# Two mixtures of experts behind an attention: rounds of 256 gathered tokens in place of slots of 128 sorted ones, and a result that stays in sorted order

## What is computed

```python
logits = xn @ en.T / tau                      # x and expert embeddings, normalised
expert_idx = np.argmax(logits, axis=1)
gate_w = probs[np.arange(N), expert_idx]      # softmax of logits, at the chosen expert
for e in range(8):                            # first mixture, w1[e] 512x1024, w2[e] 1024x512
    mask = expert_idx == e
    h = np.maximum(x[mask] @ w1[e], 0.0)
    out[mask] = gate_w[mask, None] * (h @ w2[e])
# second mixture, on that out; p = domain_probs / its row sum
for e in range(4):
    h = np.maximum(x @ w1[e], 0.0)
    out += p[:, e:e + 1] * (h @ w2[e])
```

## Time and profile before

| | us |
|---|---|
| three runs | 908.07, 909.2, 913.29 |
| median | 909.2 |
| profiled execution, its own time | 910.04 |
| its span (first to last instruction) | 908.2 |
| mean granted TensorE clock | 0.987 |

### The profile page before, as it was taken

The page is one execution under the profiler, slowest core; times in us unless marked ns, Lnnn a source line. Parts: engine busy times, 40 slices in busy tenths (PEclk is TensorE's granted clock), DMA queues, the critical chain, the costliest instruction groups (busy, mean ns, idle before and its releaser), DMA issues.

```text
span 908.2 us, 12900 instructions
## 1 busy us (share of the span) xinstructions
PE 860.9 (95%) x4433; PEld 695.1 (77%) x4434; DVE 300.3 (33%) x776; ACT 221.3 (24%) x476; POOL 288.8 (32%) x162
## 2 busy tenths in 40 slices
PE   7999945999999999999999999999999999999998
PEld 5666623788888788788888888888888888888886
DVE  6777770444444443223121212121212121211212
ACT  4878750033333323311111111111111111111010
POOL 4462613057777778630000650000830001400000
PEclk9999976999999999999999999999999999999999
DMA  6899623146666667620000230000320000001001
GB/s 246 265 315 342 221 78 140 31 124 213 205 204 205 195 220 220 174 94 1 1 0 0 70 116 0 0 0 0 115 71 0 0 0 0 1 0 46 29 17 46
DMA packets 33075, 90.96 MB, mean 100 GB/s; under 512 B 4232, under 2 KB 4616, under 8 KB 33040
## 3 DMA queue, kind: packets, MB, share of 16 engines
q1 hardware_dynamic: 23056, 54.86, 18.1%
q10 hardware_dynamic: 8064, 29.36, 10.6%
q0 software_dynamic: 1920, 6.29, 2.2%
HBM read 72.67 MB, written 17.83 MB: 100 GB/s over the span
## 4 chain that ended last, share of the span: by engine, by line
PE 84%; DMA 8%; DVE 3%; issue 2%; POOL 2%; SPq 1%; ACT 1%; DVEq 0%; ACTq 0%
PE ps L1209 29%; PE ps L1196 29%; PE ps L1153 10%; PE ps L1135 7%; DMA win<-qkv 3%; DMA xg<-x_sorted 3%; PE ps L1008 2%; PE ps L1034 2%; PE ps L1020 2%; POOL x_sorted L473 1%; PE ps L1143 1%; PE ps L1125 1%; PE ps L979 1%; PE ps L1048 1%; ACT arena L528 1%
## 5 line engine op out<-in xcount | busy, mean ns | idle before, releaser
L1209 PE MATMUL ps<-ring,h 128*128 128x512 f32 x1152 | 275.9, 390 | 0.0
L1196 PE MATMUL ps<-ring 128*128 (+1 forms) x864 | 256.4, 389 | 0.0
L278 POOL TENSOR_TENSOR ring<-raw,ring 128x1024 fp32r<-128x1024 f32 x96 | 227.9, 2403 | 84.0 <-ACT ring L273 81.1
L1209 PEld LDWEIGHTS ps<-ring,h 128*128 128x128 f32 x1152 | 215.6, 188 | 44.6
L1196 PEld LDWEIGHTS ps<-ring 128*128 128x128 f32 x864 | 162.1, 188 | 34.0 <-DVE x2b L940 0.2
L947 DVE SCALAR_TENSOR_TENSOR h<-ps,h 128x512 fp32r<-128x512 f32 x96 | 66.3, 691 | 366.3 <-ACT h L597 366.3
L597 ACT ACTIVATE h<-ps 128x512 fp32r<-128x512 f32 x96 | 57.6, 600 | 427.3 <-PE ps L1196 427.3
L273 POOL CAST ring<-raw 128x1024 fp32r<-128x1024 f32 x36 | 38.0, 1055 | 374.8 <-PE ps L1196 320.3
L1196 PE MATMUL ps<-x2b,ring 128*128 (+1 forms) x288 | 112.0, 389 | 0.0
L273 ACT CAST ring<-raw 128x1024 fp32r<-128x1024 f32 x60 | 62.2, 1051 | 176.9 <-PE ps L1153 116.7
L1135 PE MATMUL ps<-ring,xT 128*128 x384 | 91.8, 395 | 0.6 <-DVE xT L900 0.6
(11 more groups left out here) (116 smaller groups left out, 490.2 us busy)
## 6 DMA issues: line engine op xcount, KB each, us to landing
raw<-wts ACTq DMA_DIRECT2D x56, 512.0 KB, 4.2
raw<-wts SPq DMA_DIRECT2D x40, 512.0 KB, 3.8
win<-qkv SPq DMA_DIRECT2D x32, 320.0 KB, 4.1
x_sorted<-ring SPq DMA_DIRECT2D x20, 256.0 KB, 4.9
xg<-x_sorted SPq DMA_DIRECT2D x17, 256.0 KB, 3.4
y_sorted<-yrow SPq DMA_DIRECT2D x16, 256.0 KB, 4.0
win<-qkv SPq DMA_DIRECT2D x8, 384.0 KB, 6.3
result<-xrow SPq DMA_DIRECT2D x12, 256.0 KB, 2.1
```

The lines of the kernel that those rows point to most:

```text
L278: nc.gpsimd.tensor_tensor(w_part(u, 1)[:, q * CW:q * CW + CW], raw[:, q, :], w_part(u, 0)[:, q * CW:q * CW + CW].bitcast(F32), ALU.subtrac ...
L1196: ins = nc.tensor.matmul(ps[:, 4 + f % 2, :], w_part(u1, wp)[:, k * F + f * P:k * F + f * P + P], x2T(xp, k)[:, bass.ds(g * 512, 512)], st ...
L1209: ins = nc.tensor.matmul(ps[:, t, :], h2[:, f % 2, hp_, t * P:t * P + P], w_part(u1 + 1, wp)[:, f * DM:f * DM + DM], start=(f == 0 and n = ...
```

## The change

It touches nearly everything behind the attention, and a little of it.

- **Weights.** One expert is now held at a time, in 8 quarters of `ring` (two blocks f of w1 or of w2 each), and a quarter is overwritten as soon as the expert before has used it. GpSimd splits 6 quarters during attention. From there on ScalarE makes the high parts of the first mixture and of the second's first expert, GpSimd the low parts; for the second's other experts GpSimd makes both, now spread over the last group of the expert before.
- **Attention.** No zeros are stored. The squares of x leave both pipelines; ScalarE does all 12 after its pipeline. SyncE stores each finished tile of `xrow` to `x_rows`. The start is reordered a little (tau first; the flag is read ahead of the mask; idle matmuls).
- **Routing.** `find_tokens` finds, for each expert, its first 256 tokens: ranks as before, then 12 matmuls of a comparison of ranks with 0 to 127 against the one-hot rows times the token's number. Two gathers of 128 rows then bring the first round.
- **Bookkeeping.** Counts, places of the rounds, order of the tokens, gates in sorted order, and rounds beyond the eighth (experts with more than 256 tokens) are computed by VectorE in small pieces beside the first two rounds, once with 12 matmuls on TensorE (`find_order`), and SyncE stores and re-reads a table of indices.
- **First mixture.** A loop over rounds of 256 tokens of one expert. Both products have weights as the stationary operand and 256 tokens as columns, so that nothing is transposed in between and the result is already the second mixture's operand `x2T`.
- **Second mixture.** Tokens stay in sorted order. `group` has the same matmuls in another order. The result is scattered to its rows by GpSimd.

```diff
-            for u in range(PRE):
-                for q in range(4):
...
-                    high_part(pool, u, q, nc.gpsimd.tensor_copy)
-                    low_part(pool, u, q)
-            pool.wait_ge(pos_ready, 1)
-
+            for j in range(FILLED):
+                pool.wait_ge(raw_ready[j], 16)
+                nc.gpsimd.tensor_copy(ring[:, j, 0, :], raw[:, j, :]).then_inc(high_pool, 1)
+                pool.wait_ge(high_pool, j + 1)
+                low_part(j, split_done)
...
+            with pool.Fori(1, last) as c:
+                lows(c, FILLED, NQ)
+                lows(c + 1, 0, 4)
+
+                pool.wait_ge(idx_next, c + 1)
+                lows(c + 1, 4, 5)
+                gather(idx_now)
+                lows(c + 1, 5, FILLED)
...
             for t in range(NT):
+                pool.wait_ge(acc_done, (E2 - 1) * NT + t + 1)
                 nc.gpsimd.indirect_dma_start(
...
+                    out=out, out_offset=bass.IndirectOffsetOnAxis(ap=tokd[:, t:t + 1], axis=0),
+                    in_=acc[:, t, :], in_offset=None).then_inc(out_stored, 16)
```

TensorE, rounds of the first mixture:

```diff
+            def hidden(p, f):
+
+                if f % 2 == 0:
+                    pe.wait_ge(split_done, p * NQ + (NQ + f + 1))
+                if f == 0:
+                    pe.wait_ge(x_split, p * 2 + 4)
                 for k in range(KD):
...
+                    for n, (wp, xp) in enumerate(((0, 0), (0, 1), (1, 0))):
+                        ins = nc.tensor.matmul(ps[:, 4 + f % 2, 0:CH], w1(wp, f, k),
+                                               x1T[:, xp * KD + k, bass.ds(((p + 1) & 1) * CH, CH)],
+                                               start=(k == 0 and n == 0), stop=(k == KD - 1 and n == 2))
                 ins.then_inc(h_ready, 1)
...
+            def project(p, f):
+
+                pe.wait_ge(h_split, p * KF + (KF + f + 1))
+                if f % 2 == 0:
+                    pe.wait_ge(split_done, p * NQ + (NQ + f + 2))
+                for d in range(KD):
+                    if f == 0 and d % 2 == 0 and not (isinstance(p, int) and p < 0):
+                        pe.wait_ge(y_split, p * 2 + (d // 2 + 1))
+                    for n, (wp, hp_) in enumerate(((0, 0), (0, 1), (1, 0))):
+                        ins = nc.tensor.matmul(ps[:, d // 2, (d % 2) * CH:(d % 2) * CH + CH], w2(wp, f, d * P, P),
+                                               hT[:, f % 4, hp_, :], start=(f == 0 and n == 0 and d % 2 == 0),
+                                               stop=(f == KF - 1 and n == 2 and d % 2 == 1))
+                ins.then_inc(projected, 1)
...
+            def chunk(p, final=False, beside=None):
                 for f in range(KF):
                     if f + 1 < KF:
...
+                        hidden(p, f + 1)
+                    elif final:
+                        hidden2(0, 0, 0)
+                    else:
+                        hidden(p + 1, 0)
+                    if not final and f in (3, 4):
+                        turn_x(p + 1, f - 3)
+                    if beside and f == beside[0]:
+                        beside[1]()
+                    project(p, f)
```

TensorE, a group of the second mixture:

```diff
+            def group(e, g, banks_free=None):
+
+                def may_project(f):
+                    pe.wait_ge(hid_split, (g + 3 * e) * KF + (f + 1))
+                    if f % 2 == 0:
+                        pe.wait_ge(split2_done, NQ * e + f + 2)
+
+                for f in range(KF - 2):
+                    hidden2(e, g, f + 1)
+                    may_project(f)
+                    if f == 0 and banks_free:
+                        banks_free()
+                    for t in range(4):
+                        ins = project2(e, g, f, t)
+                    ins.then_inc(hid_used, 1)
+                hidden2(e, g, KF - 1)
+                may_project(KF - 2)
+                may_project(KF - 1)
+                for t in range(4):
+                    ins = project2(e, g, KF - 2, t)
+                    if t == 3:
+                        ins.then_inc(hid_used, 1)
+                    project2(e, g, KF - 1, t).then_inc(y2_ready, 1)
```

VectorE beside the first two rounds, and in each round:

```diff
+            def next_indices(c):
+
+                nc.vector.tensor_copy(idx_now[:, :], idx_all[:, bass.ds(c * 2, 2)]).then_inc(idx_next, 1)
...
+            chunk(-1, beside={1: [token_rounds], 2: [token_offsets], 3: [token_homes],
+                             4: [gate_logits], 5: [lambda: spot(lanes, 0, homes_ready, [0])], 6: [gates],
+                             7: [lambda: spot(lanes, 0, homes_ready, [1])]})
+            hidden_part(0, 0)
+            y_low_part(0)
+            chunk(0, beside={1: [gate_parts], 2: [lambda: pack(0)], 3: [lambda: pack(1)], 4: [number_extras],
+                             5: [choose_extras], 6: [read_order, read_extras], 7: [write_tables]})
...
+            with dve.Fori(1, prev) as p:
+                hidden_part(p, 0)
+                y_low_part(p)
+                dve.wait_ge(idx_more, 16 * 2 * (CHUNKS - E))
+                chunk(p)
```

More of the change, by code:

```diff
@@ new lines, in lows @@
+            def lows(c, first, end):
+                for j in range(first, end):
+                    pool.wait_ge(high_act, c * NQ + (j - FILLED + 1))
+                    low_part(j, split_done)
+            pool.wait_ge(x_stored, 16 * NT)
+            pool.wait_ge(idx_ready, 1)
+            gather(idx_all[:, 0:2])
+            pool.wait_ge(xT_psum, 2)
+            gather(idx_all[:, 2:4])
+            lows(0, FILLED, NQ)
+            lows(1, 0, 4)
+            pool.wait_ge(idx_next, 1)
+            lows(1, 4, 5)
@@ new lines, in _ @@
+            gather(idx_now)
+            lows(1, 5, FILLED)
+            pool.wait_ge(count_ready, 1)
+            prev = pool.value_load(last_i[0:1, :], min_val=E - 2, max_val=CHUNKS - 2)
+            last = prev + 1
+            with pool.Fori(1, last) as c:
[3 more added lines that the diff above has]
+                lows(c + 1, 4, 5)
+                gather(idx_now)
+                lows(c + 1, 5, FILLED)
+            for h in range(2):
+                pool.wait_ge(gathered[h], last * 16 + 32)
@@ L943, in hidden_low @@
[L943 to L951 removed]
+                find_tokens()
@@ new lines, in find_order, with chunk @@
+            def find_order():
+                pe.wait_ge(homes_ready, 2)
+                pe.wait_ge(packs_ready, 2)
+                for t in range(NT):
+                    ins = nc.tensor.matmul(ps[:, 2, 0:NT * 14], lanes[:, t, :],
+                                           packs[:, t, :, :].rearrange("p r v -> p (r v)"),
+                                           start=(t == 0), stop=(t == NT - 1))
+                ins.then_inc(homes_found, 1)
+            def chunk(p, final=False, beside=None):
@@ new lines, in _ @@
+            keep_busy(32)
+            turn_x(-1, 0)
+            turn_x(-1, 1)
+            hidden(-1, 0)
+            chunk(-1)
+            chunk(0, beside=(5, find_order))
+            pe.wait_ge(count_ready, 1)
+            prev = pe.value_load(last_i[0:1, :], min_val=E - 2, max_val=CHUNKS - 2)
+            with pe.Fori(1, prev) as p:
+                chunk(p)
+            chunk(prev, final=True)
+            pe.wait_ge(order_found, 1)
+            group(0, 0, lambda: pe.wait_ge(y_split, prev * 2 + 4))
```

1047 lines of the change are left out of this document (557 added, 490 removed).

## The result

The changed kernel takes 905.06 us (median of 6, 904.27 to 906.29), the kernel before on the same chip 911.88: a ratio of 0.9937, 95% interval 0.9918 to 0.9956. So it is faster by 0.6%, 6.8 us, where 25 were forecast. The profiled execution took 905.01 us around a span of 903.2. First the windows view of the changed kernel, with the columns of the earlier trace rows and cut at the same events: last row of x, first hidden matmul, end of the first mixture, last projection. The first hidden piece of the second mixture, 2.7 us, now lies ahead of the third cut.

The account below looks back on a forecast made before the run. TensorE, busy 860.9 of 908.2 us, was taken as the bound: its idle stretches and its instructions' number and pace. Terms -9.5 - 17.6 - 1.9 - 15.4 + 17.4 + 1.4 = -25.6 gave 884 us, range 866 to 900 (864 to 907 with two rivals).

Parts of the forecast that it names:

- A: Attention, up to the last row of x, 123.95 us before: 9.5 us less, bounds -3 to -12.
- B: From the last row of x to the first hidden matmul: 33.1 to 15.5 us, -17.6, bounds 13.5 to 20.
- TensorE's idle matmuls stand inside the two waits: Between routing and first hidden matmul: 16 and 32 idle matmuls fit inside TensorE's waits, with no time added for them.
- C: First mixture: 205.9 to 204 us, -1.9; eight rounds 191, plus one-time costs of 9 and 4.
- Before the third round's activations VectorE waits: First mixture, once: wait for SyncE to store the token order and read back ten index columns; 4 us, bounds 0 and 8.
- 4.5 us of delay in each of the two rounds: First mixture's first two rounds: VectorE's bookkeeping may end only with GpSimd's instructions; 9 us, bounds 0 and 18.
- pace: First mixture: time per pair of weight load and 256-column matmul, taken as 0.117 us, forecast range 0.110 to 0.125.
- Rivals 1 and 3: First mixture: weight load not hidden, 1,048 us, chance 0.1; or GpSimd, not TensorE, sets the round, 930 us, chance 0.03.
- D: The turn-around between the mixtures, result to memory and gathered back: its 15.4 us go.
- E: Second mixture: 526.4 to 543.8 us, +17.4; merged waits ahead of project 6 stall TensorE 1.8 us per group, 21.6 in all.
- F: Tail: +1.4 us, a scatter by GpSimd replacing a store.
- Rival 2: First mixture: VectorE and GpSimd block each other in every round, with both one-time costs at their bounds; 900 us, chance 0.14.

## Why the prediction was wrong

The sign and the mechanisms were right, 905 lies in the range near its slow end, and the size was off by a factor of four. Step by step:

- **A** held: -9.8 for -9.5. Its inside was off in both directions: the zeros are worth 6.4 in the changed kernel, not 4.5, which leaves 3.4 for the blocked VectorE instructions and the squares, not 5. That rest is a difference; no run measures it alone, and that the whole came out within 0.3 is partly luck.
- **B** gave 2.2 us less. The step left out that after the branch TensorE stands for 3.28 us and then runs 32 idle matmuls at a low clock, 5.46 us, which end at 129.1 though the second gather is there earlier. "TensorE's idle matmuls stand inside the two waits" was wrong by the 2.3 us that the run with 12 of them shows; there the stretch is 15.5 us (114.01 to 129.53), as forecast.
- **C** is the step that failed, by 16.3 of the 20.5 us, and 13.6 of that in its two costs that occur once, 13 forecast and 26.6 measured. **"Before the third round's activations VectorE waits": 4 taken, bounds 0 and 8; 14.4 measured.** The table was taken as ready about 12 us after the order is found; it took 21.2 (188.54 to 209.72), 10.9 of it the one store of single elements, and the need came 7.6 after that point, about as forecast. The measured cost lies outside the bounds. I also named what is queued behind VectorE's wait, but not what is queued behind SyncE's: the next expert's weights, which hold the round for 9.8 us by themselves. And I left out the cold restart. **"4.5 us of delay in each of the two rounds": 9 taken, 12.2 measured** (11.2 of them the lock), none in the first round and all in the second. I had taken, where an instruction ends with one subtraction of GpSimd's, as the worst case of one instruction; it can be four subtractions. The upper bound of 18 did hold it.
- The round came out at 24.35 for 23.9, pace 0.120 for 0.117, inside the bounds: 2.7 to 3.6 us over the stage. Rivals 1 and 3 were rightly small. The prediction set against each other two rules of the Trainium skill's page "TensorE: Matmul & The Clock Gate" (sections "LDWEIGHTS (loading the stationary operand)" and "Back-to-back issue gap"), the larger of load and gap, 109 ns, or their sum; the trace, 120 ns, stands near the larger and far from the sum.
- **D** held. **E** held to 0.2 us, and both directions of the edit show it: -21.5 in that stretch when undone, +21.8 when done alone, 21.6 forecast. It was the one part in which each term came from a row of the same instruction with its own neighbours.
- **F** cost 3.9, not 1.4: GpSimd's drain and the longer issue were in no row of before that I read, and I bounded them by nothing.
- Rival 2 named the lock with 900 us and was the nearest of the rivals in time, though partly for the wrong place: 3 of its 16 us lay in the steady rounds, which lose nothing to the lock, and its 8 us for the index table were 14.4. The Trainium skill's page "SBUF — State Buffer", section "SBUF: two separate sides", has the lock held for the whole instruction. That is the right kind, but the trace goes beyond it: by the records the cast began 0.1 us before the first of the four subtractions and still ended after the fourth, 9.50 us for one instruction's lock.

So the expected gain wasn't hidden elsewhere; it was there and was given back at three waits: 19 us at the end of the groups (foreseen), 14 at the index table (foreseen at 4) and 11 at the lock (foreseen at 9).

## What to carry to other kernels

A wait that is needed in the fifth round and stands in every round is paid in the first; put it where its value is first used, and do the same on every queue that stands behind the same event, since mending VectorE's alone gave 4 us and with SyncE's 14. When costs that occur once come late in a chain (find, store, load back, then work), time the chain from its own first event to its last and set it against the time of need; a store of single 4-byte elements is a long link. Small VectorE work placed beside a GpSimd backlog can wait for all of it, and moving one instruction away only hands the wait to the next: shorten the backlog or keep the bookkeeping off the path.

## What the runs showed of the hardware that I had not expected

- A VectorE cast of 24 columns waited through four GpSimd subtractions in a row, 9.50 us; with GpSimd's instructions short it takes 0.17. By the records the cast began first (159.85 and 159.95).
- Back-to-back pairs of a float32 load and 128 columns left the granted clock at 0.50 for 240 us; with 256 columns it came back within 10 us, with 512 in the second mixture too.
- A store of 7 KB as 1,792 single elements took 10.88 us to be seen, an index column of 0.5 KB read back 2.0 (median).
- GpSimd's drain takes 2.52 us behind the last indexed store and then ends the program; where its last indexed transfer lay in the first mixture it takes 4.00 (at 764.42) and is off the path.
- Pairs of a float32 load and 128 columns are 256 cycles apart at either clock, 0.213 and 0.107 us, so at the full clock halving the columns of a pair from 256 saves 0.013 of 0.120.
